# Feeding a seven-product gate stage: the order of gating, weight casts, weight loads and PSUM banks in a fused attention and feed-forward kernel

## The reference

```python
def _attn_ref(q, k, v, tau):                    # q, k, v: 1 x 6016 x 256
    qn = q / (np.linalg.norm(q, axis=1, keepdims=True) + 1e-06)
    kn = k / (np.linalg.norm(k, axis=1, keepdims=True) + 1e-06)
    s = kn.transpose(0, 2, 1) @ qn / tau        # 256 x 256
    s = s - s.max(-1, keepdims=True)
    a = np.exp(s)
    a /= a.sum(-1, keepdims=True) + 1e-09
    return (v @ a).astype(np.float32)

def _moe_ref(x, w_gate, w_val, w_out, rms_g):   # d_ff 1536
    rms = np.sqrt(np.mean(x * x, axis=-1, keepdims=True) + 1e-06)
    xn = x / rms * rms_g
    g = xn @ w_gate
    silu = g * (1.0 / (1.0 + np.exp(-g)))
    val = xn @ w_val
    return (silu * val @ w_out).astype(np.float32)

def _moe2_ref(x, w_in, w_out):                  # d_ff 2048
    h = x @ w_in
    g = h - np.tanh(h)
    return (g @ w_out).astype(np.float32)
```

## Time and profile before

| | |
|---|---|
| median of 3 runs | 1400.82 us (1400.54 to 1401.34) |
| the profiled execution | 1402.32 us, span 1400.5 us |
| mean granted TensorE clock | 0.946 of full |
| PE busy | 1219.5 us, 87% of the span |
| DVE busy | 959.5 us, 69% |
| ACT busy | 462.9 us, 33% |
| POOL busy | 250.4 us, 18% |
| DMA | 104.83 MB, mean 75 GB/s |

### The profile page before, as it was taken

How to read it: one execution, slowest core, us unless ns; L and a number is a source line. 1 busy time by engine, 2 the same in 40 slices (tenths; PEclk the granted TensorE clock), 3 DMA queues, 4 the chain that set the end, 5 groups by cost and what they waited for, 6 DMA issues and landing times.

```text
span 1400.5 us, 18368 instructions
## 1 busy us (share of the span) xinstructions
PE 1219.5 (87%) x5858; PEld 1027.6 (73%) x5858; DVE 959.5 (69%) x1760; ACT 462.9 (33%) x775; POOL 250.4 (18%) x208
## 2 busy tenths in 40 slices
PE   9999999599869959986995998699599679899899
PEld 8888888478657847865774786587478568778798
DVE  6878878468647836954783695577468458678666
ACT  8756233134224213322321331242133124233222
POOL 5500010230131023013102301310220140130120
PEclk9999999889989979998997999899799989999999
DMA  9333640420140032014003202301320330230200
GB/s 372 116 120 76 165 151 1 121 91 1 45 133 32 7 112 90 0 47 133 30 17 103 90 0 56 124 30 41 86 83 0 74 132 0 75 110 12 76 31 12
DMA packets 132790, 104.83 MB, mean 75 GB/s; under 512 B 90640, under 2 KB 112784, under 8 KB 132752
## 3 DMA queue, kind: packets, MB, share of 16 engines
q1 hardware_dynamic: 132320, 103.83, 24.0%
q10 hardware_dynamic: 432, 0.52, 0.1%
HBM read 91.88 MB, written 12.45 MB: 74 GB/s over the span
## 4 chain that ended last, share of the span: by engine, by line
PE 66%; DVE 10%; DMA 8%; issue 6%; POOL 4%; SPq 3%; ACT 2%; DVEq 0%; ACTq 0%
PE ring L1497 28%; PE out_acc L1557 17%; PE y_acc L1557 8%; DMA landing<-combined 7%; PE ring L1550 5%; DVE h_lo L1256 3%; POOL wl L718 3%; SPq L536 2%; PE out_acc L1481 2%; PE ring L1513 2%; POOL act L725 2%; PE y_acc L1418 1%; SPq L558 1%; DVE act L1212 1%; DVE gate_pair L1202 1%
## 5 line engine op out<-in xcount | busy, mean ns | idle before, releaser
L838 ACT ACTIVATE act<-ring 128x512 f32<-128x512 f32 (+1 forms) x273 | 160.9, 590 | 344.9 <-PE ring L1497 317.5
L1497 PE MATMUL ring<-y_hi,wl 128*128 128x512 f32 (+1 forms) x712 | 241.2, 385 | 0.0
L1557 PE MATMUL out_acc<-h_hi,wl 128*128 128x512 f32 x704 | 240.0, 389 | 0.4 <-DVE h_lo L1256 0.3
L1256 DVE TENSOR_TENSOR h_lo<-act,h_hi 128x512 fp32r<-128x512 f32 (+1 forms) x336 | 234.0, 709 | 8.0
L1550 PE MATMUL ring<-t_parts,wl 128*128 128x256 f32 (+1 forms) x660 | 108.1, 297 | 131.3 <-DVE act L1169 131.3
L718 POOL CAST wl<-landing 128x1024 fp32r<-128x1024 f32 x120 | 130.4, 1116 | 442.9 <-DMA landing<-combined 442.9
L725 POOL TENSOR_TENSOR act<-gate_pair,act 128x512 f32<-128x512 f32 (+1 forms) x60 | 80.7, 1345 | 635.5 <-ACT act L875 635.5
L1550 PEld LDWEIGHTS ring<-t_parts,wl 128*128 128x128 f32 x660 | 92.6, 201 | 137.0 <-DVE act L1169 137.0
L1175 DVE TENSOR_TENSOR act<-ring,act 128x512 f32<-128x512 f32 (+1 forms) x192 | 128.8, 671 | 55.9 <-ACT act L838 55.0
L1557 PEld LDWEIGHTS out_acc<-h_hi,wl 128*128 128x128 f32 x704 | 132.1, 188 | 28.7 <-DVE h_lo L1256 0.7
L1497 PEld LDWEIGHTS ring<-y_hi,wl 128*128 128x128 f32 x712 | 133.5, 188 | 25.6
(11 more groups left out here) (232 smaller groups left out, 2057.6 us busy)
## 6 DMA issues: line engine op xcount, KB each, us to landing
landing<-combined SPq DMA_DIRECT2D x60, 1024.0 KB, 5.4
out_dram<-out_rows SPq DMA_DIRECT2D x88, 64.0 KB, 1.8
qk_in<-in_k_dram SPq DMA_DIRECT2D x9, 512.0 KB, 9.1
qk_in<-in_q_dram SPq DMA_DIRECT2D x9, 512.0 KB, 9.8
v_in<-in_v_dram SPq DMA_DIRECT2D x72, 64.0 KB, 2.3
w_in<-in_moe_w_out_dram SPq DMA_DIRECT2D x12, 256.0 KB, 3.0
combined<-wl SPq DMA_DIRECT2D x12, 256.0 KB, 4.3
combined<-w_in SPq DMA_DIRECT2D x12, 256.0 KB, 3.2
```

Source lines behind the costliest of these rows:

```text
L838: nc.scalar.activation(act[:, u % RING, 0:width], bank(t, name)[:, 0:width], func).then_inc(act_ready, 1)
L1256: nc.vector.tensor_tensor(h_lo[:, u % RING, 0:width], act[:, u % RING, 0:width], f32(h_hi[:, u % RING, 0:width]), ALU.subtract).then_inc(h ...
L1497: ins = nc.tensor.matmul(bank(t, name)[:, 0:width], weights(c, w_part), (hi if part else lo)[:, c, 0:width], start=c == 0 and w_part and part,
L1557: ins = nc.tensor.matmul(acc[:, d, 0:width], weights, (h_hi if part else h_lo)[:, u % RING, 0:width], start=f == 0 and w_part and part, st ...
```

## The change

Four edits, all for tiles 2 to 11. They alter order, waits and bank assignment; the arithmetic and the number of instructions stay.

- POOL: the casts of the next block stand one pair later, behind the gating of the next pair.
- SP: blocks 3, 4 and 5 are loaded together, ahead of the loads of v.
- DVE: in odd units up to f = 9 both multiplications stand ahead of `seven_value`; for p below 3 the two low parts stand behind all seven steps.
- PSUM: LAST_THREE no longer write over `own`. For p of 4 and above gate0, gate1 and value0 go over sum1, sum2 and sum3; below, gate0 and gate1 go to `y_acc` and value0 over sum2. The waits of `free_bank`, of LAST_THREE and of the first down projection follow.

```diff
-        LAST_THREE = (("own", 1, (1, 0)), ("sum1", 5, (1, 1)), ("sum2", 3, 3))
+        LAST_THREE = (("gate0", 1, (1, 0)), ("gate1", 5, (1, 1)), ("value0", 3, 3))
...
-            if p < LAG and name != "own":
-                return y_acc[:, 0 if name == "sum1" else 1, :]
-            return bank(t, (name, p))
+            if p < LAG and name != "value0":
+                return y_acc[:, 0 if name == "gate0" else 1, :]
+            return bank(t, (LAST_OVER[p < LAG][name], p))
+
+        LAST_OVER = ({"gate0": "sum1", "gate1": "sum2", "value0": "sum3"}, {"value0": "sum2"})
+
+        FIRST_LEFT = {"sum2": BY_U2, "sum1": BY_U4, "sum3": BY_VALUE1}
+        LAST_LEFT = {"gate0": BY_GATE0, "gate1": BY_GATE1, "value0": BY_VALUE0}
...
                 store(t - 1, TILE)
-                load_sevens(t, LOADS)
+                for j in range(LOADS, 2 * LOADS):
+                    load_sevens(t, j)
                 sp.wait_ge(v_turned, t)
                 load_v(t + 2, TILE)
-                for j in range(LOADS + 1, 2 * LOADS):
-                    load_sevens(t, j)
...
-            for t in range(SEVEN_FROM, TILES):
-                for j in range(SEVENS):
-                    gate_seven(t, 2 * j)
-                    ahead = j + len(SEVEN_BLOCKS)
-                    if t < TILES - 1 or ahead < SEVENS:
-                        mark_seven(t + ahead // SEVENS, ahead % SEVENS)
+            MARKED = len(SEVEN_BLOCKS)
+            for n in range(SEVENS * (TILES - SEVEN_FROM)):
+                gate_seven(SEVEN_FROM + n // SEVENS, 2 * (n % SEVENS))
+                if n > 0:
+                    ahead = n - 1 + MARKED
+                    if ahead < SEVENS * (TILES - SEVEN_FROM):
+                        mark_seven(SEVEN_FROM + ahead // SEVENS, ahead % SEVENS)
...
-                low()
-                dve.wait_ge(seven_full, sevens(t, p, PRODUCTS, OWN_LAST))
+                if p >= LAG:
+
+                    low()
+                dve.wait_ge(seven_full, sevens(t, p, PRODUCTS, GATE0))
...
+                if p < LAG:
+                    low()
...
-                        gate_times(t, f, buf, width, lambda: seven_value(t, f - 1, width))
-                        if f == G - 1:
+                        ending = f == G - 1
+                        if ending:
+                            gate_times(t, f, buf, width, lambda: seven_value(t, f - 1, width))
                             low_unit(t, f - 1, width)
+                        else:
+                            gate_times(t, f, buf, width)
+                            seven_value(t, f - 1, width)
...
+                elif left[0] == "own":
+                    pe.wait_ge(own_copied, sevens(t, left[1], 1, 1))
                 else:
-                    pe.wait_ge(seven_step, sevens(t, left[1], STEPS, steps_taken(left[1], left[0])))
+                    pe.wait_ge(seven_step, sevens(t, left[1], STEPS, steps_left(left[1], left[0])))
...
-                        elif name == "own":
-                            pe.wait_ge(own_copied, sevens(t, p, 1, 1))
-                        elif p >= LAG:
-                            pe.wait_ge(seven_step, sevens(t, p, STEPS, BY_U4 if name == "sum1" else BY_U2))
+                        elif name in LAST_OVER[p < LAG]:
+                            pe.wait_ge(seven_step, sevens(t, p, STEPS, FIRST_LEFT[LAST_OVER[p < LAG][name]]))
```

More of the change, by code:

```diff
@@ L484, in build, with steps_left @@
         FIRST_FOUR = (("own", 0, (0, 0)), ("sum2", 4, 1), ("sum3", 6, 2), ("sum1", 7, 0))
-        LAST_THREE = (("own", 1, (1, 0)), ("sum1", 5, (1, 1)), ("sum2", 3, 3))
-        OWN, SUM2, SUM3, SUM1, OWN_LAST, SUM1_LAST, SUM2_LAST = range(1, 8)
+        LAST_THREE = (("gate0", 1, (1, 0)), ("gate1", 5, (1, 1)), ("value0", 3, 3))
+        OWN, SUM2, SUM3, SUM1, GATE0, GATE1, VALUE0 = range(1, 8)
         PRODUCTS, STEPS, T_STEPS = 7, 8, 4
-        BY_U2, BY_U4, BY_VALUE1, BY_GATE0, BY_GATE1, BY_VALUE0 = 1, 3, 4, 5, 6, 7
-        def seven_bank(t, p, name):
-            return bank(t, (name, p))
+        BY_U2, BY_U3, BY_U4, BY_VALUE1, BY_GATE0, BY_GATE1, BY_VALUE0 = range(1, 8)
         def last_bank(t, p, name):
-            if p < LAG and name != "own":
-                return y_acc[:, 0 if name == "sum1" else 1, :]
[L499 to L509, removed]
+            if p < LAG and name != "value0":
[4 more added lines that the diff above has]
+        LAST_LEFT = {"gate0": BY_GATE0, "gate1": BY_GATE1, "value0": BY_VALUE0}
+        def steps_left(p, name):
+            for last, over in LAST_OVER[p < LAG].items():
+                if over == name:
+                    return LAST_LEFT[last]
+            return FIRST_LEFT[name]
         def store_rows(eng, b, made, count):
@@ L633, in _ @@
             store(1, TILE)
-            load_sevens(SEVEN_FROM, LOADS)
+            for j in range(LOADS, 2 * LOADS):
+                load_sevens(SEVEN_FROM, j)
             sp.wait_ge(v_turned, 2)
             load_v(4, TILE)
-            for j in range(LOADS + 1, 2 * LOADS):
-                load_sevens(SEVEN_FROM, j)
             with sp.Fori(SEVEN_FROM + 1, TILES - 3) as t:
@@ L1199, in seven_sums @@
                 nc.vector.tensor_tensor(value1, of("sum3"), gate1, ALU.add).then_inc(seven_step, 1)
-                low()
-                dve.wait_ge(seven_full, sevens(t, p, PRODUCTS, OWN_LAST))
[L1202 to L1206, removed]
+                if p >= LAG:
+                    low()
+                dve.wait_ge(seven_full, sevens(t, p, PRODUCTS, GATE0))
+                nc.vector.tensor_tensor(gate0, last_of("gate0"), gate0, ALU.add).then_inc(seven_step, 1)
+                dve.wait_ge(seven_full, sevens(t, p, PRODUCTS, GATE1))
+                nc.vector.tensor_tensor(gate1, last_of("gate1"), gate1, ALU.add).then_inc(seven_step, 1)
+                dve.wait_ge(seven_full, sevens(t, p, PRODUCTS, VALUE0))
+                nc.vector.tensor_tensor(value0, last_of("value0"), value0, ALU.add).then_inc(seven_step, 1)
+                if p < LAG:
+                    low()
             def seven_value(t, p, width):
@@ L1541, in seven_products @@
                         else:
-                            pe.wait_ge(seven_step, sevens(t, p - 2, STEPS, BY_VALUE0))
-                        to = (last_bank if last else seven_bank)(t, p, name)
+                            pe.wait_ge(seven_step, sevens(t, p - 2, STEPS, BY_GATE1))
+                        to = last_bank(t, p, name) if last else bank(t, (name, p))
                         for w_part, part in PASSES:
@@ L1666, in tile @@
                                 if not is_plain(t):
-                                    pe.wait_ge(seven_step, sevens(t, LAG - 1, STEPS, BY_VALUE0))
+                                    pe.wait_ge(seven_step, sevens(t, LAG - 1, STEPS, BY_GATE1))
                         down("down", late, late, G, y_acc, y_full)
```

## The result

| | before | after |
|---|---|---|
| median | 1401.0 us (1400.54 to 1401.34, 4 runs) | 1223.6 us (1223.24 to 1223.82, 4 runs) |
| span of the profiled execution | 1400.5 us | 1221.4 us |
| PE busy / idle in the span | 1219.5 / 181.0 us | 1179.6 / 41.8 us |
| mean granted clock | 0.946 | 1.00 |
| DVE, ACT, POOL busy | 959.5, 462.9, 250.4 us | 963.3, 455.1, 262.1 us |

The ratio is 0.8734 (95% interval 0.8719 to 0.8749). Of the 179.1 us that the span lost, 139.2 are idle time of PE and 39.9 are PE's busy time, with the same 5858 matmuls: the clock. The time lies 4.4 us under the range (1228 to 1294); the direction and the mechanism were as forecast, the sizes of what remains were not.

The account below looks back on a forecast made before the run. PE's idle time in ten gate stages was the bound. A stage of 50.2 + 6.5 + 0.8 = 57.5 us, not 74.3, saves 134 us in eight, plus 4 and 3: 1402.3 less 141 is 1261, median 1260; range 1228 to 1294.

Parts of the forecast that it names:

- The long waits: PE's waits in pairs 4 and 6 of gate stages, caused by POOL's and SP's orders, would go; eight are 98 us.
- The load is hidden: In gate stages block 4, loaded early, arrives with some 8 us to spare: 0 us, or 0 to 2 if slower.
- rival C: Gate-stage block loads land late or v is held, so the load stays on the path: 1340 us, chance 0.03.
- Banks: PE's 38.6 us of waits before odd units' gate products go; gate0 of LAST_THREE waits for the third step instead.
- The port: DVE and POOL slowing each other in SBUF: 2.2 us a gate stage, contained in the forecast waits; upper end 3.8 more.
- What is late next: Waits left to PE in a changed gate stage, from pair 0 to the tail: sum 6.5 us.
- the walk: Hand count of DVE, ACT and PE through one gate stage with profiled durations; it gave PE's waits, 6.5 us.
- The loop: In gate stages, one pair's first step to the next's: 8.2 us against PE's 7.9, so DVE and ACT bound.
- Clock: In gate stages, one stretch at the lower granted clock, 1.75 us, in half the tiles: 0.8 us a stage.
- Tile 10: Its gate stage falls from 60.8 to 57 us, a gain of 4 us.
- Tile 11: Its gate stage, 384 wide, 8.6 of 51.9 us idle, gains 3 us; narrower DVE work bounds it as well.
- Rival A: The walk is too pessimistic: PE keeps under 3.5 us idle in a gate stage, about 1225 us, chance 0.15.

## Why the prediction missed its range

*The long waits.* Right, and for the stated reason: the two ties in POOL's and SP's orders. Undoing either brings its load's wait back (block 3's cast starts 16.1 us into a stage, block 4's 31.3), and both orders alone give 1398.97 less 1243.52, 155 of the 177 us.

*The load is hidden.* Right. Block 4 needs no wait of POOL; rival C is out.

*Banks.* The waits for own's bank go and gate0's wait for the third step comes, as said. The banks are worth 13 us alone, 20 behind the other orders (1243.5 to 1223.4) and 69 with DVE's order present. That DVE's order needs the new banks, and adds nothing to them, I had not seen.

*The port.* For `seven_value` the mechanism and, in sum, the size were right: the six of a stage take 1.9 us more than 6 x 0.68, where 2.2 were budgeted, though only two of them are over 1.0 us. In five of the six pairs POOL's cast has begun first, but both multiplications stand ahead of `seven_value`, so that it waits only 0.1 to 0.7 us, and not for a whole cast, which would have made the 38 us that the prediction weighed. Taking these meetings away gave 11.0 us, 1.1 a stage, since part of them lies beside PE's work. What the budget lacked is POOL's gating of pair 2: the two low parts of units 0 and 1 now stand beside it and take 2.42 us (653.68 above; 2.38 to 2.42 in tiles 2 to 10), where the two of pair 4 take 1.28. With POOL's old order, where that gating comes 7 us later, the same two take 1.28 as well (at 677.31). By the rows this 1.1 us goes through `seven_value` and the copy straight into pair 4's third step, and so into PE's wait of 0.84 us there. That is argued and not tested: with POOL's casts held back both stay as they are (2.42 and 0.84).

*What is late next.* This is the step that failed: "Sum 6.5 us", the waits left to PE in a stage. They measure 4.2 us. The places were right in pairs 2 to 8 and the tail, the sizes were not. The last row counts the same waits by the hole in PE's issue, as explained below:

| | pair 2 | pair 4 | pair 6 | pair 8 | pair 10 | tail | sum |
|---|---|---|---|---|---|---|---|
| forecast | 1.7 | 1.2 | 1.3 | 0.9 | 0.5 | 0.9 | 6.5 |
| measured | 1.19 | 0.84 | 1.01 | 0.55 | 0 | 0.61 | 4.2 |
| by issue | 1.5 | 1.0 | 1.2 | 0.7 | 0.2 | 0.8 | 5.4 |

A part of the 2.3 us is probably a double count. A matmul of 512 columns lasts 0.39 us in the profile while the next is issued after 0.225, so a wait counted from when PE could have issued is some 0.16 us longer than the profile's, which begins when the last matmul ends. The prediction says that it counts "as the profile would count them". If the walk in fact counted by issue, its sum was added to 50.2 us of work that already holds these ends, 1.2 us over the seven waits. The other 1.1 us are 0.1 to 0.3 us too much in each column: handovers were taken as 0.1 and from DVE to PE are 0.06 (L1206 ends at 653.76, PE starts at 653.82), and in pair 10 the hole is 0.2 us and the profile shows no wait. The loop itself was well sized: from the first step of pair 8 (677.25) to that of pair 10 (685.57) it takes 8.32 us, the port's 0.2 in it, against a forecast of 8.2. That the excess was in the sum and not in the loop is worked out from these rows. No run isolates the double count, and the walk itself is in no row, so how the 2.3 us divide stays open.

*Clock.* "1.75 us, in half the tiles ... 0.8": measured 0. The granted clock is 1.00 in all gate stages. With waits of 0.87 and 0.32 us between pair 0 and f = 3 no stretch followed in any tile; with 0.5, 1.2 and 2.1 us there (old banks, new orders) one did in some stages and not in others.

Together the stage is 57.5 − 54.5 = 3.0 us shorter than forecast, times 8 is 24 us. *Tile 10*: 8.2 us gained, not 4. *Tile 11*: 10.3 us, not 3; I had guessed that the narrower DVE work would bind, and did not walk it. DVE is busy for 39.09 of 41.60 us there, but PE's idle time fell from 8.6 to 1.1 us, and its busy time by 2.9, which is clock and stood in no term of mine. The eight stages before were on average 0.25 us longer than the one I took, 2 us. 24 + 4 + 7 + 2 = 37 us, which is the miss within the rounding (1260 − 1223.6 is 36.4). Rival A, the walk is too pessimistic, comes nearest: its price of 1225 was met, but by luck. Its condition, under 3.5 us idle in a stage, was not (4.2), its reason was another, and tiles 10 and 11 and the clock made up for it.

## What to carry to other kernels

An instruction that waits for a late transfer holds everything behind it in its queue. List for each in-order queue which waits nobody behind them needs, and move those back: here two such moves, with not one instruction less, were worth 155 of 177 us. When a forecast adds waits from a hand walk to work read from a trace, both must count a wait from the same moment: here the two ways of counting differ by 1.2 us in a stage. Edits that each look harmless depend on one another: DVE's order cost 49 us with the old banks and nothing with the new.

## What the runs showed of the hardware

A DVE instruction with both inputs in SBUF that becomes ready just behind the start of a POOL cast of 128 x 1024 takes 1.34 to 1.50 us in place of 0.68 (`seven_value` in the changed kernel and with DVE's old order), and one that comes later in the first of the two casts 0.81 to 0.88 (tiles 2 to 9); POOL's pair of casts takes 2.48 in place of 2.02. With DVE's old order `seven_value` starts earlier and takes 1.41 us in five of six pairs; with that and the waits for the value's bank the kernel gained nothing (1223.43 against 1223.60 us). The multiplication at L1167, with one input in PSUM, stays at 0.69 us beside a cast (683.04, the cast running from 682.94).

The same waits of PE gave different clocks in stages of one run. With POOL's and SP's orders alone the gate stages of tiles 2 to 9 are in turn at 0.97 and 1.00, each with waits of about 0.5, 0.5 and 2.1 us up to f = 3, and take about 57.2 and 55.6 us. In the changed kernel, whose longest wait is 1.01 us, every stage is at 1.00.
